# Experts' second product with w2 stationary and 512 tokens of h moving, with reversed columns in three experts

## What is computed

```python
p = domain_probs / (domain_probs.sum(-1, keepdims=True) + 1e-09)
out = np.zeros((N, D))                      # N = 3072, D = 384, F = 1024
for e in range(4):
    h = np.maximum(x @ w1[e], 0.0)          # N x F
    out += p[:, e:e + 1] * (h @ w2[e])      # N x D
```

## Time and profile before

| | |
|---|---|
| median of 3 runs | 1219.05 us (1218.25 to 1219.37) |
| span of the profiled execution | 1217.6 us |
| TensorE busy | 1212.3 us, 7740 matmuls |
| VectorE busy | 461.4 us |
| ScalarE busy | 281.7 us |
| GpSimd busy | 168.8 us |
| DMA, mean | 89 GB/s |

### The profile page before, as it was taken

The page is one execution under the profiler, slowest core; times in us unless marked ns, Lnnn a source line. Parts: engine busy times, 40 slices in busy tenths (PEclk is TensorE's granted clock), DMA queues, the critical chain, the costliest instruction groups (busy, mean ns, idle before and its releaser), DMA issues.

```text
span 1217.6 us, 18865 instructions
## 1 busy us (share of the span) xinstructions
PE 1212.3 (100%) x7740; PEld 1118.6 (92%) x7740; DVE 461.4 (38%) x886; ACT 281.7 (23%) x526; POOL 168.8 (14%) x148
## 2 busy tenths in 40 slices
PE   9999999999999999999999999999999999999998
PEld 8799999999999999999999999999999999999998
DVE  6997586586651122122222222222122222222222
ACT  3443333333333311111111111111111111111111
POOL 1132222222223520000000000000000000000000
PEclk9999999999999999999999999999999999999999
DMA  9644444544415331100141111123101111222201
GB/s 286 207 121 122 126 132 106 137 128 105 126 47 195 106 145 52 51 17 36 53 156 52 52 52 52 52 73 135 42 15 46 52 52 53 78 78 78 78 9 44
DMA packets 87543, 108.03 MB, mean 89 GB/s; under 512 B 38576, under 2 KB 57904, under 8 KB 86960
## 3 DMA queue, kind: packets, MB, share of 16 engines
q1 hardware_dynamic: 87184, 106.63, 28.0%
q10 hardware_dynamic: 288, 0.39, 0.1%
HBM read 86.29 MB, written 18.35 MB: 86 GB/s over the span
## 4 chain that ended last, share of the span: by engine, by line
PE 99%; DVE 0%; issue 0%; DVEq 0%; ACT 0%
PE bank L1175 33%; PE bank L1294 25%; PE bank L1022 9%; PE bank L1024 9%; PE bank L1023 9%; PE score_banks L1294 8%; PE bank L1063 2%; PE bank L1244 1%; PE score_banks L1084 1%; PE bank L1073 1%; PE score_banks L1047 1%; PE bank L1226 1%; PE bank L1214 0%; DVE total L1000 0%; PE bank L1031 0%
## 5 line engine op out<-in xcount | busy, mean ns | idle before, releaser
L821 DVE SCALAR_TENSOR_TENSOR h_lo<-bank,h_hi 128x512 fp32r<-128x512 f32 x192 | 132.8, 691 | 584.9 <-ACT h_hi L601 584.0
L601 ACT ACTIVATE h_hi<-bank 128x512 fp32r<-128x512 f32 x192 | 114.7, 597 | 661.7 <-PE bank L1175 661.7
L1175 PE MATMUL bank<-x_hi,we_lo 128*128 128x512 f32 x576 | 228.7, 397 | 0.0
L1175 PE MATMUL bank<-x_hi,we_hi 128*128 128x512 f32 x576 | 224.1, 389 | 0.0
L1175 PE MATMUL bank<-x_lo,we_hi 128*128 128x512 f32 x576 | 223.5, 388 | 0.0
L1294 PE MATMUL bank<-we_hi,h_hi 128*128 128x384 f32 x576 | 194.6, 338 | 0.0
L1294 PE MATMUL bank<-we_lo,h_hi 128*128 128x384 f32 x576 | 194.5, 338 | 0.0
L1294 PE MATMUL bank<-we_hi,h_lo 128*128 128x384 f32 x576 | 193.8, 336 | 0.0
L499 POOL TENSOR_TENSOR we_lo<-we_raw,we_hi (+1 forms) x48 | 60.9, 1289 | 527.8 <-ACT we_hi L562 527.8
L1175 PEld LDWEIGHTS bank<-x_hi,we_lo 128*128 128x128 f32 x576 | 108.3, 188 | 22.4
L1175 PEld LDWEIGHTS bank<-x_lo,we_hi 128*128 128x128 f32 x576 | 108.0, 188 | 22.7
(11 more groups left out here) (99 smaller groups left out, 1473.3 us busy)
## 6 DMA issues: line engine op xcount, KB each, us to landing
x_hi<-x_hi_spill SPq DMA_DIRECT2D x24, 768.0 KB, 4.8
x_lo<-x_lo_spill SPq DMA_DIRECT2D x24, 768.0 KB, 6.3
we_raw<-wset SPq DMA_DIRECT2D x4, 3072.0 KB, 10.0
inputs<-akq SPq DMA_DIRECT2D x24, 448.0 KB, 5.2
values<-v_rows SPq DMA_DIRECT2D x24, 256.0 KB, 3.7
inputs<-akq SPq DMA_DIRECT2D x24, 224.0 KB, 3.3
x_hi_spill<-x_hi_out SPq DMA_DIRECT2D x8, 576.0 KB, 4.3
x_lo_spill<-x_lo_out SPq DMA_DIRECT2D x8, 576.0 KB, 5.2
```

Of the source, the lines that this page charges most:

```text
L601: act.activation(h_hi[:, s % 2, :], bank[s % 2][:, :], ACT.Relu).then_inc(h_hi_ready, 1)
L821: dve.scalar_tensor_tensor(out=h_lo[:, s % 2, :], in0=bank[s % 2][:, :], scalar=0.0, in1=h_hi[:, s % 2, :], op0=ALU.max, op1=ALU.subtract) ...
L1175: mm = pe.matmul(bank[s % 2][:, :], (we_hi if term < 2 else we_lo)[e % 2][:, cols], (x1_lo if term == 1 else x1_hi)[u][:, k, :], start=(i ...
```

## The change

In the experts' down product the operands change places. w2 is stationary, in three blocks of 128 output columns, and 512 tokens of h move: 9 matmuls of 512 columns a step in place of 12 of 384. The result is transposed (output column over partitions, token along the free axis). So `total` and the output are too, and the host turns the output back. `step2` alternates one down and one up, nine times.

The share of a token now varies along the free axis, so it is no longer a scalar of a partition. The gates are stored to DRAM once, and for each expert read back as a row that is copied to all 128 partitions (`gate_rows`, 128x3072, two buffers). `add` multiplies each of three banks by that row: into `total` for expert 0, into `shares` for the others, followed by three additions to `total` (`summed`). GpSimd's clearing of `total` is gone. The sums have two sets of three banks, one for each tile of a round.

Last, the tokens' order: `UP_COLUMNS` and `DOWN_COLUMNS` give for each expert the direction in which the columns of the moving operand are read and those of the bank written. Expert 0: all forward. Expert 1: x read and h's bank written backward. Expert 2: x read backward and h's bank written forward, so that h lies reversed; h is then read backward and its sum written forward. Expert 3: h read and its sum written backward. The results are the same.

```diff
@@ -53,7 +53,6 @@
-SUBS = TILE2 // P
@@ -64,9 +63,11 @@
-SUM_BANKS = [5, 2, 3, 4]
+FORWARD, BACKWARD = slice(None), slice(None, None, -1)
+UP_COLUMNS = [(FORWARD, FORWARD), (BACKWARD, BACKWARD), (BACKWARD, FORWARD), (FORWARD, FORWARD)]
+DOWN_COLUMNS = [(FORWARD, FORWARD), (FORWARD, FORWARD), (BACKWARD, FORWARD), (BACKWARD, BACKWARD)]
+SUM_BANKS = [[5, 6, 7], [2, 3, 4]]
...
-assert KT * TERMS == SUBS * TERMS - TERMS
@@ -89,6 +90,7 @@
+    gate_dram = nc.dram_tensor("gate_spill", [EXPERTS, TOKENS], F32, kind="Internal").ap()
@@ -107,7 +109,7 @@
-        gate = sb("gate", [P, TOKENS // P, EXPERTS])
+        gate = sb("gate", [P, EXPERTS, TOKENS // P])
@@ -182,7 +184,9 @@
-        total = sb("total", [P, TOKENS // P, DM])
+        total = sb("total", [P, KT, TOKENS])
+        gate_rows = [sb(f"gate_rows{i}", [P, TOKENS]) for i in range(2)]
+        shares = sb("shares", [P, KT, TILE2])
@@ -262,19 +266,21 @@
-        total_zero = sem("total_zero")
+        gate_stored = sem("gate_stored")
+        gate_rows_loaded = [sem(f"gate_rows_loaded{i}") for i in range(2)]
...
+        summed = sem("summed")
...
-        ADDED_AHEAD = SUBS
+        ADDED_AHEAD = 2 * KT
@@ -369,6 +375,9 @@
+
+            def load_gate_rows(e):
+                sp.dma_start(gate_rows[e % 2][:, :], gate_dram[e:e + 1, :].to_broadcast([P, TOKENS])).then_inc(gate_rows_loaded[e % 2], 16)
@@ -441,6 +450,8 @@
+            sp.dma_start(gate_dram.rearrange("e (p t) -> p e t", p=P), gate[:, :, :]).then_inc(gate_stored, 16)
@@ -459,23 +470,27 @@
+            sp.wait_ge(gate_stored, 16)
+            load_gate_rows(0)
...
-                    sp.wait_ge(down_done, SUBS * TILES2 * e)
+                    sp.wait_ge(down_done, KT * TILES2 * e)
+                    sp.wait_ge(added, ADDED_AHEAD + KT * TILES2 * e)
...
+                    load_gate_rows(e + 1)
...
-                        count = 1 if tile + 1 == TILES2 else SUBS
-                        for i in range(0, SUBS, count):
-                            sp.wait_ge(added, ADDED_AHEAD + SUBS * n + i + count)
-                            at = slice(tile * SUBS + i, tile * SUBS + i + count)
-                            sp.dma_start(out[:, at, :], total[:, at, :]).then_inc(stored, 16)
-            sp.wait_ge(stored, 16 * (TILES2 - 1 + SUBS))
+                        count = 1 if tile + 1 == TILES2 else KT
+                        for i in range(0, KT, count):
+                            sp.wait_ge(summed, KT * (n - TILES2) + i + count)
+                            at = slice(tile * TILE2, (tile + 1) * TILE2)
+                            sp.dma_start(out[:, i:i + count, at], total[:, i:i + count, at]).then_inc(stored, 16)
+            sp.wait_ge(stored, 16 * (TILES2 - 1 + KT))
@@ -537,8 +552,6 @@
-            pool.wait_ge(x1_final, 1)
-            pool.memset(total[:, :, :], 0.0).then_inc(total_zero, 1)
@@ -991,14 +1004,15 @@
-                dve.wait_ge(total_zero, 1)
-                for i in range(SUBS):
-                    dve.wait_ge(down_done, SUBS * n + i + 1)
-                    t = (2 * m + u) * SUBS + i
-                    sum_so_far = total[:, bass.ds(t, 1), :].rearrange("p a d -> p (a d)")
-                    share = gate[:, bass.ds(t, 1), e:e + 1].rearrange("p a d -> p (a d)")
-                    dve.scalar_tensor_tensor(out=sum_so_far, in0=bank[SUM_BANKS[i]][:, 0:DM], scalar=share, in1=sum_so_far,
-                                             op0=ALU.mult, op1=ALU.add).then_inc(added, 1)
+                at = bass.ds((2 * m + u) * TILE2, TILE2)
+                dve.wait_ge(gate_rows_loaded[e % 2], 16 * (e // 2 + 1))
+                for i in range(KT):
+                    dve.wait_ge(down_done, KT * n + i + 1)
+                    dve.tensor_tensor(total[:, i, at] if e == 0 else shares[:, i, :], bank[SUM_BANKS[u][i]][:, :], gate_rows[e % 2][:, at],
+                                      ALU.mult).then_inc(added, 1)
+                for i in range(KT if e else 0):
+                    dve.wait_ge(added, ADDED_AHEAD + KT * n + i + 1)
+                    dve.tensor_tensor(total[:, i, at], total[:, i, at], shares[:, i, :], ALU.add).then_inc(summed, 1)
@@ -1172,7 +1185,8 @@
-                mm = pe.matmul(bank[s % 2][:, :], (we_hi if term < 2 else we_lo)[e % 2][:, cols], (x1_lo if term == 1 else x1_hi)[u][:, k, :],
+                read, written = UP_COLUMNS[e]
+                mm = pe.matmul(bank[s % 2][:, written], (we_hi if term < 2 else we_lo)[e % 2][:, cols], (x1_lo if term == 1 else x1_hi)[u][:, k, read],
@@ -1284,14 +1298,14 @@
-                sub, term = divmod(i, TERMS)
-                if term == 0 and e == 0 and s == 0 and sub >= 1:
-                    pe.wait_ge(x1_lo_ready, X1_LOW_AHEAD + KT * (TILES1 * BATCH - 1) + sub)
+                part, term = divmod(i, TERMS)
...
-                    pe.wait_ge(added, SUBS * (e * TILES2 + 2 * m + u) + sub + 1)
-                rows = slice(sub * P, (sub + 1) * P)
-                cols = slice(KT * FF + f * DM, KT * FF + (f + 1) * DM)
-                mm = pe.matmul(bank[SUM_BANKS[sub]][:, 0:DM], (h_hi if term < 2 else h_lo)[:, s % 2, rows], (we_lo if term == 1 else we_hi)[e % 2][:, cols],
+                    if e == 0 and u == 1 and part == 0:
+                        pe.wait_ge(x1_lo_ready, X1_LOW_AHEAD + KT * TILES1 * BATCH)
+                    pe.wait_ge(added, KT * (e * TILES2 + 2 * m + u) + part + 1)
+                cols = slice(KT * FF + f * DM + part * P, KT * FF + f * DM + (part + 1) * P)
+                read, written = DOWN_COLUMNS[e]
+                mm = pe.matmul(bank[SUM_BANKS[u][part]][:, written], (we_hi if term < 2 else we_lo)[e % 2][:, cols], (h_lo if term == 1 else h_hi)[:, s % 2, read],
@@ -1301,12 +1315,10 @@
-                ups = 0
-                for i in range(SUBS * TERMS):
+                for i in range(KT * TERMS):
...
-                    if ahead and i % SUBS >= 1:
-                        up2_product(ahead[0], ahead[2], ups)
-                        ups += 1
+                    if ahead:
+                        up2_product(ahead[0], ahead[2], i)
@@ -1367,15 +1379,15 @@
-    out = nc.dram_tensor("out", [P, TOKENS // P, DM], F32, kind="ExternalOutput").ap()
+    out = nc.dram_tensor("out", [P, KT, TOKENS], F32, kind="ExternalOutput").ap()
...
-    return np.ascontiguousarray(result.transpose(1, 0, 2)).reshape(TOKENS, DM)
+    return np.ascontiguousarray(result.transpose(2, 1, 0)).reshape(TOKENS, DM)
```

More of the change, by code:

```diff
@@ L443, in _ @@
             load_set(1)
+            sp.wait_ge(gate_steps, 5)
+            sp.dma_start(gate_dram.rearrange("e (p t) -> p e t", p=P), gate[:, :, :]).then_inc(gate_stored, 16)
             sp.wait_ge(x0_moved, MOVED * BATCH * CHUNKS)
@@ L842, in scale_gate @@
                 dve.wait_ge(gate_loaded, 16)
-                dve.tensor_reduce(gate_sum[:, :], gate[:, :, :], AX.X, ALU.add).then_inc(gate_steps, 1)
+                dve.tensor_reduce(gate_sum[:, :], gate[:, :, :].rearrange("p e t -> p t e"), AX.X, ALU.add).then_inc(gate_steps, 1)
                 dve.wait_ge(gate_steps, 2)
@@ L848, in scale_gate @@
                 dve.wait_ge(gate_steps, 4)
-                dve.tensor_tensor(gate[:, :, :], gate[:, :, :], gate_inv[:, :, None].to_broadcast([P, TOKENS // P, EXPERTS]),
+                dve.tensor_tensor(gate[:, :, :], gate[:, :, :], gate_inv[:, None, :].to_broadcast([P, EXPERTS, TOKENS // P]),
                                   ALU.mult).then_inc(gate_steps, 1)
@@ L1010, in _ @@
             dve.sem_inc(added, ADDED_AHEAD)
-            dve.wait_ge(gate_steps, 5)
             for e in range(EXPERTS):
@@ L1369 @@
         "wset0": wset0,
-        "probs": by_rows(moe2_domain_probs),
+        "probs": np.ascontiguousarray(moe2_domain_probs.reshape(P, TOKENS // P, EXPERTS).transpose(0, 2, 1)),
     }
```

## The result

The change makes the kernel slightly slower: 1223.18 us against 1219.09 (medians of 6 runs each), a ratio of 1.0035 with a 95% interval of 1.0025 to 1.0045. Forecast were 1228.7 and "slower", so the sign was right and the size more than twice too large. The profiled execution of after took 1225.42 us, 2.2 over its own median; its span is 1223.7.

The account below looks back on a forecast made before the run. TensorE's matmul starts were taken as the bound, all else counting only where TensorE waits. On a 1217.6 us span, 7.5 + 0 + 0 + 0 + 2.1 = +9.6 gave 1227.2, a median of 1228.7 us; range 1205 to 1240.5.

Parts of the forecast that it names:

- Part 1, the products: Experts' interleaved steps: 18 matmuls of 512 columns at 233.3 ns, 4.200 us a step against 4.161, +7.5 us.
- 512-only run: Nine ups ahead of the first down, before the change: 233.3 ns each after the first two, taken for all 18.
- the further 6.7 ns: Extra cost of an up in the experts' stream, not shown on the first after shorter matmuls, partly absorbed by those between.
- rival (a): Experts' stream: fixed cost a matmul, 226.7 ns at 512, 1205.9 us; if half escape, 4.140 a step, 1217.2; chance 0.18.
- Part 2, the reversed orders: Experts 1 to 3: 1728 matmuls reading the moving operand reversed, taken as zero, bounds +11.5 and -11.5 us.
- The scan on VectorE: Nearest row for reversed reads: suffix scan, reversed, 490 ns against 518 for the forward scan; basis for taking zero.
- Rival (c): Experts 1 to 3: reversed streams pay 6.7 ns each, 1240.2 us; chance 0.12 together with a compiler split of matmuls.
- (d): Experts 1 to 3: reversed streams escape the penalty, -11.5 us, 1217.2 us; chance 0.08.
- (b): Experts' stream: cost by columns alone, 231.2 ns a matmul, 1221.4 us, the same within 0.2%; chance 0.12.
- (e): Experts: reversed orders make the compiler split a matmul, 1240.2 us or worse; chance 0.12 shared with reversed streams paying.
- parts 3, 4 and 5: VectorE adding to the total, hidden with 1.1 us spare; DMA queues, zero; the end after the last matmul, +2.1 us.
- part 4: Queues: gate_rows load delays second expert's weights 5 us, to 440; h_lo perhaps a microsecond late, hidden; zero.

Follow-up runs that it names:

- the blocks: Changed kernel, all columns forward, each step's nine downs before its nine ups: 1218.63 us; with x1 also moved 32 bytes, 1206.64 us.
- the moves: Changed kernel, all columns forward, operands shifted in memory: x1 by 32 bytes 1206.10 us; h alone to a multiple of 64 1228.45; everything at multiples of 64 1229.05.
- the opposite sequence: Changed kernel with the experts' column orders in opposite sequence (expert 0 h backward, 1 both, 2 x backward, 3 all forward): 1223.05 us, ratio 1.0036.

## Why the prediction was wrong, point by point

**Part 1, the products, is the term that failed.** It said that the 512-only run is "the nearest row" and took 233.3 ns for all 18. In the steady stream the nine ups cost 233.3 each and the nine downs 226.7, so with all forward a step is 4.140 us in place of 4.200, -3.9 us over 190 steps in place of +7.5. I had read the further 6.7 ns as a property of 512 columns after each other; the blocks and x moved by 32 bytes show that in the steady stream it hangs on where the moving operand lies. That does not explain the row that I took, though: with x moved the same run of ups still takes 231 ns each, while the stream behind it runs at 226.7. The row showed nine matmuls behind shorter ones and not a steady stream of 512 columns. That its 233.3 fits the ups of the changed kernel is luck as far as the runs show, and that it does not fit the downs no row of before could show, since in none does h move. The fault was to let such a row stand for all 18; rival (a) had the measured value, "half of the matmuls escape", 4.140 a step, without saying which half. The sentence on how the prediction would be wrong, a cost that depends on what stands beside a matmul in another way than the lone run shows, names what happened.

**Part 2, the reversed orders, was taken at zero and is not.** The bound on it was right in size, 6.7 ns a matmul, but x and h had to be kept apart: backward h costs it, 864 matmuls in experts 2 and 3 or 5.6 us by the steps (94 x 0.060), and backward x nothing, since x pays it already. The scan on VectorE was no neighbour of a read by TensorE. Rival (c), reversed streams pay, was right as a mechanism for h, on a base that was wrong; (d), reversed streams escape, had the sign wrong. (b), cost by columns, came near the number, 1221.4, and explains nothing. Rival (a)'s 226.7 for all came true once x was moved. Of (e) nothing is seen: 7164 matmuls are the 7740 of before less three a step, so none was split.

**The two errors partly cancel.** -3.9 + 5.6 = +1.7 for the steps (1.9 measured), +2.1 for the end: +3.8 against 4.1 measured. Forecast was 7.5 + 0 + 2.1.

**Right were** parts 3, 4 and 5: the end at +2.1 (2.11 in the profile), the additions 0.60 apart, h_lo with about a microsecond to spare, TensorE without a wait at a tile's edge as before, and the later weights hidden. The details of part 4: I had put the load of gate_rows at 5 us and the weights' landing at 440; it took 6.6, and they landed at about 441. The microsecond of delay that I allowed h_lo did not come.

**The chances** do not add up by their own parts: half of (b) and the rest of (d) are 0.06 + 0.02 = 0.08 for "same", where I wrote 0.12, and "slower" should have had 0.68.

**The test named in the prediction worked.** It said to compare the distances expert by expert, since the experts differ in just the orders. That one view of after separates the two errors; that the first goes by the operand and its place took the blocks and the moves.

**Still open.** Why an all-forward stream, with h 32 over a multiple of 64, sometimes runs at 233.3 for h too and then stays there. Why a stream of 384 and 512 columns costs 4.161 a step with x at a multiple of 64 and 4.240 with x moved. Why a run of nine ups behind shorter matmuls costs 231 ns each with x at either place. In all three the price hangs on what the neighbours do or did, and these runs don't show by what means.

## What to carry to other kernels

Read a matmul's cost as the distance of starts, and take it from a steady stretch with the same moving operand and the same neighbours: two operands of one shape differed by 3% by their address alone, and a short run behind shorter matmuls did not show that difference at all. Where TensorE has no idle time, try the moving operands at another offset first; in this kernel 32 bytes of padding together with one width for all matmuls brought 12.9 us; one width alone, all forward, brought 1.8 in the median (1217.31 against 1219.16), and two of its ten runs were 10 us or more slower than before. Try it on the stream as it will be, since the same 32 bytes cost the kernel before 15 us.

## What the runs showed of the hardware that I had not expected

- In a steady stream of 512-column matmuls, each with its own weight load, a forward moving operand of float32r cost 226.7 ns when it began 32 bytes over a multiple of 64 and 233.3 when it began at one; read backward from an operand 32 over it cost 233.3 (4.085 and 4.140 a step with x forward and backward). With all forward two of ten executions had the higher price for h too. Only offsets of 0 and 32 were tried, so the period may be another than 64: counted by 128, the cheap places (3552, 7648, 12000) are all 96 over, and the dear ones 0 or 64. Nine such matmuls behind matmuls of 384 columns cost 231 each at either place. The place of the weights made no difference (1229.05 and 1228.45 us), and the direction of the write none that the times show (1217.61 and 1217.31). The Trainium skill, SBUF — State Buffer, Specifications (TRN2), gives cachelines of 16 bytes; both places are multiples of 16, so that alone doesn't account for the difference.
- 226.7 is the shortest steady distance seen for 512 columns, 13.3 over the 213.3 of columns / 2.4. The Trainium skill, TensorE: Matmul & The Clock Gate, Back-to-back issue gap, gives 2.5 over for an isolated warm matmul; no stretch here came near it.
- In a steady stream a rhythm can hold for 800 us and differ from execution to execution (1217 and 1229 us with all forward), at a granted clock of 0.999 to 1.000 in every run. From 4.200 us a step it went to 4.140 where x was read backward and h forward, and stayed there when all was forward again (the opposite sequence).
- At 226.7 ns for 512 columns a column costs 0.443 ns against 0.451 at 384. So what the Trainium skill, Perfetto Trace Analysis, Optimizing Tensor Performance, Matmuls, says, that larger matmuls are more efficient, holds here once x is moved; at 233.3 it is 0.456, and it does not.
